# Attention and two mixture layers on one core: a product moved to VectorE, rows moved inside SBUF, grouped spreads

## The chip, the cores and the metric

The program runs on one core of a Trainium2 chip. The metric is the device time of one execution in microseconds (us). The engines are TensorE (PE, weight loads PEld), VectorE (DVE), ScalarE (ACT), GpSimd (POOL) and SyncE (SP, which here only issues DMAs).

## The reference, cut to what matters

```python
# B, H, S, D = 2, 8, 768, 40: attention over q, k, v with gates
m_new = np.maximum(f_gate[:, :, t] + m, i_gate[:, :, t])
C = f_stab * C + i_stab * einsum('bhd,bhe->bhde', vt, kt)
n = f_stab * n + i_stab * kt
y[:, :, t] = sigmoid(o_gate[:, :, t]) * einsum('bhde,bhe->bhd', C, qt) / maximum(abs(n . qt), 1)
# x = y as (1536, 320) rows, then a dense layer
h = x @ w_in                       # 320 -> 2048
g = maximum(h, 0) + log1p(exp(-abs(h)))
x = g @ w_out                      # 2048 -> 320
# then each token goes through its best one of 8 experts
h = maximum(x[mask] @ w1[e], 0); out[mask] = gate_w * eom * (h @ w2[e])
```

## The kernel before, in words

The order of the work is written out by hand: each engine has a block of its own with waits on semaphores, and every DMA but the gates' second half, the token fetches and the results is issued by SP, in one order.

**Attention, 16 heads in 8 pairs.** Time is cut into 6 chunks of 128 steps. For pair j (batch 0 is pairs 0 to 3, batch 1 pairs 4 to 7) TensorE broadcasts gate rows over the partitions (`cast`, L1382), computes the scores of keys and queries within a chunk (`scores`, L1407), the state updates of each chunk from `kw` and `v1` (`updates`, L1421), and the outputs, first from weighted scores `p_w` and `v1`, then from the states and `qd` (`outputs`, L1435). ScalarE copies casts out of PSUM (L803) and the finished pair to `stage` (L820). VectorE scans the forget gates over 768 steps, once per head (`scan`, L1071), scans the states (`states`, L1081), and multiplies scores by the decay (`weigh`, L1092). GpSimd makes `v1` = v times input gate (`inputs`, L610), `kw` = k times decay (`keys`, L622) and `qd` = q times decay (`queries`, L632). `v1` has 2 buffers, `kq` (keys and queries, 40 + 40 partitions) 3.

**Between attention and the dense layer.** A finished pair is stored to HBM (`store_pair`, L380: two times 40 rows to `attn_rows`, two normaliser rows to `nq_rows`). For batch 0 the rows come back early, heads 0 to 5 after pair 2 (`load_early`, L388), the rest after pair 3 (`load_late`, L396): `den` is the normaliser, 48 numbers to each partition, `xn` the output rows in three tiles of 128 partitions (tile 2 holds the last 64 rows twice). VectorE computes 1/max(|n.q|, 1) (`normaliser`, L1094); SP stores it to `rden_rows` and spreads it with one broadcast DMA for each piece of a head (`spread_normaliser`, L421) to `rb`. Then the tiles are multiplied by the output gate (`first_gate` L1103 on VectorE, `output_gate` L635 on GpSimd) and by `rb` (`normalise`, L1108), and split in a high part `xhi` (ScalarE, `high_part`, L827) and a low part `xlo` (VectorE, L1118). On VectorE the gate and `normalise(0)` stand between `states(6)` and `weigh(7)`.

**Dense layer, two batches of 16 tiles.** Each tile of `w_in` is loaded (L440), split in high and low on VectorE (`high_in`, L1139) and GpSimd (`split_in`, L668), multiplied in `hidden` (L1514: per half, for each 128 rows of x, high by high, high by low, low by high), goes through the softplus on ScalarE (L886) and VectorE (`gate_tile`, L1150), and through `second` (L1535). The first `hidden` waits for each tile's high and low part in turn. Batch 1's rows take the same way through HBM while batch 0's dense tiles run: its normaliser is spread after the third pair of tile loads (L503), in one queue with the loads of w_in and w_out. Afterwards come routing and the experts; the change does not touch them.

```python
for k, at, first, n in NORM_PIECES:
    if first_head <= first < last_head:
        sp.dma_start(rb[at:at + n, k, :], rden_rows[H * b + first:H * b + first + 1, :].to_broadcast([n, S])).then_inc(loaded, 16)
```

Of the kernel before, what the change touches and what calls it, by code (L numbers as in the profile page):

```python
# [6 lines left out]
ALU = mybir.AluOpType  # L7
# [8 lines left out]
P = 128  # L16
B, H, S, D = 2, 8, 768, 40
HEADS = B * H
NC = S // P
# [25 lines left out]
CONSTS = 17  # L45
# [21 lines left out]
NORM_PIECES = norm_pieces()  # L67
LATE_PIECES = sum(first >= EARLY for _, _, first, _ in NORM_PIECES)
EARLY_PIECES = len(NORM_PIECES) - LATE_PIECES
# [28 lines left out]
def build_program(nc, kq_t, k_rows, v_rows, o_t, gates, w_in, w_out, w_out_t, route_w, w1_e, w2_e, out):  # L98
    ctx = ExitStack()
    with ctx:  # L100
# [35 lines left out]
        need_k = keep.place("need_k", [P, TT], F32)  # L136
        table = keep.place("table", [P, TABLES, SLOTS + 1], I32)
# [19 lines left out]
        pick_1 = gat.place("pick_1", [P, HEADS], F32)  # L157
        assert gat.at <= after_x
# [17 lines left out]
        route_t = early.place("route_t", [P, F1 // 4], F32)  # L176
# [7 lines left out]
        v1 = [att.place(f"v1{u}", [P, 2 * NC, V1], F32) for u in range(2)]  # L184
# [81 lines left out]
        attn_rows = nc.dram_tensor("attn_rows", [HEADS * D, S], F32, kind="Internal").ap()  # L266
        nq_rows = nc.dram_tensor("nq_rows", [HEADS, S], F32, kind="Internal").ap()
# [16 lines left out]
        q_zeroed = sem("q_zeroed")  # L284
# [38 lines left out]
        block = ctx.enter_context(nc.Block())  # L323

# [39 lines left out]
        def _(sp):  # L364
            def load_kq(j):
                if j >= 3:
                    sp.wait_ge(scores_ready, j - 2)
                    sp.wait_ge(qd_done, j - 2)
                for h in range(2):
                    sp.dma_start(kq[j % 3][HALF * h:HALF * h + D, :, :], kq_t[2 * j + h].rearrange("d (k t) -> d k t", k=2)).then_inc(kq_loaded[j % 3], 16)  # L370
# [17 lines left out]
            def load_early():  # L388

                sp.wait_ge(stage_stored[0], 96)  # L390
                sp.wait_ge(stage_stored[1], 48)
                sp.dma_start(den[0:16 * EARLY, 0, :], nq_rows[0:EARLY, :].rearrange("h (p n) -> (h p) n", n=NQ)).then_inc(nq_early, 16)
                sp.dma_start(xn[:, 0, :], attn_rows[0:P, :]).then_inc(xn_early, 16)
                sp.dma_start(xn[0:EARLY * D - P, 1, :], attn_rows[P:EARLY * D, :]).then_inc(xn_loaded, 16)

            def load_late():  # L396

                sp.wait_ge(stage_stored[1], 96)
                sp.dma_start(den[16 * EARLY:P, 0, :], nq_rows[EARLY:H, :].rearrange("h (p n) -> (h p) n", n=NQ)).then_inc(nq_loaded, 16)
                sp.dma_start(xn[EARLY * D - P:P, 1, :], attn_rows[EARLY * D:2 * P, :]).then_inc(xn_loaded, 16)  # L400
                for at in (0, HALF):
# [1337 lines left out]
```

## Time and profile before

| what | us |
|---|---|
| median of 3 runs (420.04 to 422.71) | 420.82 |
| the profiled execution | 417.85 |
| its span, from the first to the last instruction | 416.1 |
| TensorE busy | 386.2 (93%) |
| VectorE busy | 283.7 (68%) |
| ScalarE busy | 225.9 (54%) |
| GpSimd busy | 212.2 (51%) |

The span is the profiled execution without its start and end. A timeline row gives start, duration, engine, line, operation, tiles and shapes, a count where several were merged, and in brackets the idle time before it and what ended that.
### The profile page before, as it was taken

How to read it: one execution, taken by the hardware profiler on the slowest of the kernel's cores; microseconds unless marked ns; L12 is line 12 of the kernel's file. 1: busy time of each engine (PE TensorE's matmuls, PEld its weight loads, DVE VectorE, ACT ScalarE, POOL GpSimd, SP SyncE). 2: the span in 40 equal slices, each digit the busy share in tenths (PEclk: the TensorE clock that was granted, in tenths of full speed). 3: DMA queues.
4: the chain of work that ended last, by engine and by line, in shares of the span. 5: the costliest groups of instructions: out<-in, count | busy, mean ns of one | idle time of the engine just before them, and what ended most of it. 6: DMA issues, size and time to landing. Idle time of an engine off the chain costs nothing.

```text
span 416.1 us, 9463 instructions
## 1 busy us (share of the span) xinstructions
PE 386.2 (93%) x2741; PEld 359.5 (86%) x2742; DVE 283.7 (68%) x496; ACT 225.9 (54%) x406; POOL 212.2 (51%) x225
## 2 busy tenths in 40 slices
PE   0999996899999999999999999599999999999983
PEld 0858886789999999999999999588998999899873
DVE  8999989958656788557766676677473257874231
ACT  4647772454556545655555655546465358874230
POOL 6577978436556665342434464045264423886221
PEclk9999997899999999999999999989999999999998
DMA  7979774335255544644222254225736219741110
GB/s 198 304 286 320 231 221 147 112 83 165 76 182 172 184 134 153 189 135 166 72 71 61 66 202 143 105 64 174 277 117 260 64 40 354 262 153 36 56 36 26
DMA packets 30682, 63.43 MB, mean 152 GB/s; under 512 B 8984, under 2 KB 20763, under 8 KB 30012
## 3 DMA queue, kind: packets, MB, share of 16 engines
q1 hardware_dynamic: 28780, 57.61, 42.6%
q0 software_dynamic: 1808, 5.31, 3.8%
q8 instruction: 14, 0.23, 0.2%
q10 hardware_dynamic: 64, 0.15, 0.1%
q14 instruction: 16, 0.13, 0.1%
HBM read 56.40 MB, written 6.88 MB: 152 GB/s over the span
## 4 chain that ended last, share of the span: by engine, by line
PE 83%; DVE 8%; issue 2%; DMA 2%; ACT 2%; DVEq 0%; POOL 0%; SPq 0%; POOLq 0%; ACTq 0%
PE ps L1541 7%; PE ps L1543 7%; PE ps L1542 7%; PE ps L1525 5%; PE ps L1527 5%; PE ps L1526 5%; PE ps L1674 4%; PE ps L1676 4%; PE ps L1675 4%; PE ps L1631 3%; PE ps L1633 3%; PE ps L1632 3%; PE ps L1658 3%; PE ps L1532 3%; PE ps L1533 3%
## 5 line engine op out<-in xcount | busy, mean ns | idle before, releaser
L1156 DVE SCALAR_TENSOR_TENSOR gsum<-ps,soft 128x384 f32<-128x384 f32 x64 | 35.7, 557 | 51.8 <-ACT soft L897 51.5
L670 POOL TENSOR_TENSOR win_lo<-win_raw,win_hi 128x256 fp32r<-128x256 f32 x32 | 25.1, 783 | 85.6 <-DVE win_hi L1143 85.6
L889 ACT ACTIVATE soft<-ps 128x384 f32<-128x384 f32 x64 | 31.5, 492 | 68.5 <-PE ps L1533 68.4
L1541 PE MATMUL ps<-wout_hi,ghi 128*128 128x336 f32 x192 | 61.1, 318 | 1.0 <-DVE glo L1162 1.0
L1542 PE MATMUL ps<-wout_lo,ghi 128*128 128x336 f32 x192 | 60.7, 316 | 0.0
L1543 PE MATMUL ps<-wout_hi,glo 128*128 128x336 f32 x192 | 60.7, 316 | 0.0
L1525 PE MATMUL ps<-xhi,win_hi 128*128 128x384 f32 x128 | 43.6, 341 | 0.8 <-DVE gsum L1156 0.8
L1527 PE MATMUL ps<-xhi,win_lo 128*128 128x384 f32 x128 | 43.3, 338 | 0.0
L1526 PE MATMUL ps<-xlo,win_hi 128*128 128x384 f32 x128 | 43.2, 338 | 0.0
L1674 PE MATMUL ps<-split,hthi 128*128 x120 | 38.3, 319 | 1.9 <-DVE htlo L1333 1.9
L737 POOL DMA_INDIRECT out<-yout,token x15 | 17.7, 1177 | 41.3 <-DVE yout L1341 40.3
L1541 PEld LDWEIGHTS ps<-wout_hi,ghi 128*128 128x128 f32 x192 | 36.1, 188 | 1.8 <-issue 1.2
L1676 PE MATMUL ps<-split,htlo 128*128 x120 | 37.1, 309 | 0.0
L1675 PE MATMUL ps<-split,hthi 128*128 x120 | 37.0, 308 | 0.0
L1542 PEld LDWEIGHTS ps<-wout_lo,ghi 128*128 128x128 f32 x192 | 36.2, 189 | 0.0
L1543 PEld LDWEIGHTS ps<-wout_hi,glo 128*128 128x128 f32 x192 | 36.2, 188 | 0.0
L710 POOL TENSOR_TENSOR split<-e2raw,split (+1 forms) x16 | 26.4, 1667 | 18.6 <-ACT split L946 15.7
L1159 DVE CAST ghi<-gsum 128x384 fp32r<-128x384 f32 x64 | 34.1, 575 | 0.0
L897 ACT ACTIVATE soft<-soft 128x384 f32<-128x384 f32 x64 | 33.4, 521 | 1.0
L893 ACT ACTIVATE soft<-soft 128x384 f32<-128x384 f32 x64 | 33.3, 521 | 1.0
L1071 DVE TENSOR_TENSOR_SCAN d_w<-f_all,ident 128x768 f32<-128x768 f32 x16 | 32.5, 2071 | 0.4 <-ACT f_all L803 0.3
L1162 DVE TENSOR_TENSOR glo<-gsum,ghi 128x384 fp32r<-128x384 f32 x64 | 32.5, 548 | 0.0
(214 smaller groups left out, 996.2 us busy)
## 6 DMA issues: line engine op xcount, KB each, us to landing
e1raw<-w_e SPq DMA_DIRECT2D x24, 512.0 KB
e2raw<-w_e SPq DMA_DIRECT2D x16, 640.0 KB, 5.2
win_raw<-w_in SPq DMA_DIRECT2D x32, 192.0 KB, 2.6
wout_raw<-w_out SPq DMA_DIRECT2D x32, 160.0 KB, 2.1
kq<-kq_t SPq DMA_DIRECT2D x16, 240.0 KB
wout_t<-w_out_t SPq DMA_DIRECT2D x3, 1024.0 KB, 14.1
og<-o_t SPq DMA_DIRECT2D x2, 1152.0 KB, 7.4
kr<-k_rows SPq DMA_DIRECT2D x8, 240.0 KB, 4.7
```

Of the source, the lines that this page charges most:

```text
L897: nc.scalar.activation(soft_half(f, hf), soft_half(f, hf), ACT.Ln, bias=1.0).then_inc(ln_done, 1)
L1156: dve.scalar_tensor_tensor(half(gsum, hf), ps[:, hf, 0:S // 2], 0.0, half(soft, hf), ALU.max, ALU.add).then_inc(g_done, 1)
L1159: dve.tensor_copy(half(ghi[u], hf), half(gsum, hf)).then_inc(ghi_done, 1)
L1525: pe.matmul(o, hi[:, k, :], xhi[b][:, k, cols], start=(k == 0), stop=False)
L1526: pe.matmul(o, hi[:, k, :], xlo[b][:, k, cols], start=False, stop=False)
L1527: pe.matmul(o, lo[:, k, :], xhi[b][:, k, cols], start=False, stop=False)
L1541: pe.matmul(o, ghi[u][:, cols], wout_hi[u][:, :], start=False, stop=False, skip_group_check=True)
L1542: pe.matmul(o, ghi[u][:, cols], wout_lo[u][:, :], start=False, stop=False, skip_group_check=True)
L1543: last = pe.matmul(o, glo[u][:, cols], wout_hi[u][:, :], start=False, stop=last_tile, skip_group_check=True)
L1674: pe.matmul(o, hthi[:, k, :], w(e2hi, k), start=(k == 0), stop=False)
L1675: pe.matmul(o, hthi[:, k, :], w(e2lo, k), start=False, stop=False)
L1676: last = pe.matmul(o, htlo[:, k, :], w(e2hi, k), start=False, stop=(k == FET - 1))
```

## The change

- `queries` (qd) moves from GpSimd to VectorE, behind the two scans and ahead of `weigh`; GpSimd waits for it before `keys` and `inputs`. `v1` gets a third buffer.
- Batch 0's rows are no longer stored and loaded: `store_pair` moves the normaliser row (16 partitions of 48) into `den` and the rows into `xn`, straight from `stage` in SBUF. Batch 1 keeps the way through HBM for its rows, but not for the normaliser. `load_early` and `load_late` go.
- `spread_normaliser` takes neighbouring whole heads together in one DMA: heads 0 to 2 (120 partitions), heads 4 and 5 (80 partitions). 9 DMAs for a batch in place of 12.
- VectorE gates tiles 0 and 2 (`open_tile`), GpSimd tile 1. ScalarE makes the high part of w_in's tile 0 after pair 4 and GpSimd its low part there.
- The first dense product (`first_hidden`) takes all products with `xhi` for both halves first and those with `xlo` last.
- Of VectorE's clears at the start, two of `kq` go to ScalarE and `f_start` to GpSimd.

```diff
+def head_pieces(head):
+    pieces = []
+    first, last = head * D, head * D + D
+    for k in range(KT):
+        lo, hi = max(first, k * P), min(last, k * P + P)
+        if lo < hi:
+            pieces.append((k, lo - k * P, lo - first, hi - lo))
+            if k == KT - 1:
+                pieces.append((k, lo - k * P + REM, lo - first, hi - lo))
+    return pieces
+
+def spreads(first_head, last_head):
+    groups = []
+    for k, at, head, n in norm_pieces():
+        if first_head <= head < last_head:
+            same = groups and n == D and groups[-1][4] == D and groups[-1][0] == k and groups[-1][1] + groups[-1][3] * D == at
+            if same:
+                groups[-1] = (k, groups[-1][1], groups[-1][2], groups[-1][3] + 1, D)
+            else:
+                groups.append((k, at, head, 1, n))
+    return groups
...
-        v1 = [att.place(f"v1{u}", [P, 2 * NC, V1], F32) for u in range(2)]
+        v1 = [att.place(f"v1{u}", [P, 2 * NC, V1], F32) for u in range(3)]
...
+        def wait_stored(engine, j):
+            engine.wait_ge(stage_stored[j % 2], STORED[j])
+
+        def wait_queries(engine, j):
+            engine.wait_ge(qd_done, j + 1)
...
             def store_pair(j):
...
                 for h in range(2):
-                    sp.dma_start(attn_rows[(2 * j + h) * D:(2 * j + h + 1) * D, :], stage[u][HALF * h:HALF * h + D, :]).then_inc(stage_stored[u], 16)
-                sp.dma_start(nq_rows[2 * j:2 * j + 2, :], stage[u][D:D + HALF + 1:HALF, :]).then_inc(stage_stored[u], 16)
+                    at = 16 * (2 * j + h - H * b)
+                    sp.dma_start(den[at:at + 16, b, :], stage[u][HALF * h + D:HALF * h + V1, :].rearrange("o (p n) -> o p n", n=NQ)).then_inc(stage_stored[u], 16)
+                for h in range(2):
+                    if b == 0:
+                        for k, at, first, n in head_pieces(2 * j + h):
+                            rows = slice(HALF * h + first, HALF * h + first + n)
+                            sp.dma_start(xn[at:at + n, k, :], stage[u][rows, :]).then_inc(stage_stored[u], 16)
+                    else:
+                        sp.dma_start(attn_rows[(2 * j + h - H) * D:(2 * j + h - H + 1) * D, :], stage[u][HALF * h:HALF * h + D, :]).then_inc(stage_stored[u], 16)
...
-                for k, at, first, n in NORM_PIECES:
-                    if first_head <= first < last_head:
-                        sp.dma_start(rb[at:at + n, k, :], rden_rows[H * b + first:H * b + first + 1, :].to_broadcast([n, S])).then_inc(loaded, 16)
+                for k, at, head, heads, n in spreads(first_head, last_head):
+                    source = rden_rows[H * b + head:H * b + head + heads, :]
+                    sp.dma_start(rb[at:at + heads * n, k, :],
+                                 source.unsqueeze(1).to_broadcast([heads, n, S])).then_inc(loaded, 16)
...
             for j in range(1, PAIRS - 1):
-                queries(j)
+                wait_queries(pool, j)
                 keys(j + 1)
                 inputs(j + 1)
+                if j == 5:
+                    split_in(0, 0)
+                    pool.wait_ge(win_split, 2)
...
             iteration(4)
+            act.wait_ge(win_loaded[0], 16)
+            nc.scalar.copy(win_hi[0][:, :, :], win_raw[0][:, :, :]).then_inc(win_hi_done, 1)
...
+            def open_tile(k):
+                for j in ((0, 1), (1, 2, 3), (3,))[k]:
+                    wait_stored(dve, j)
+                dve.wait_ge(og_ready, k + 1)
+                dve.tensor_tensor(xn[:, k, :], xn[:, k, :], og[0][:, k, :], ALU.mult).then_inc(z_first, 1)
...
                 if j == 4:
-                    normaliser(0, slice(0, 16 * EARLY), nq_early, 16, 0)
+                    normaliser(0, slice(0, 16 * EARLY), (1, 2), 0)
                 if j == 5:
-                    normaliser(0, slice(16 * EARLY, P), nq_loaded, 16, 1)
+                    normaliser(0, slice(16 * EARLY, P), (3,), 1)
+                queries(j + 1)
                 weigh(j + 1)
...
+            def first_hidden():
+                pe.wait_ge(win_split, 2)
+                pe.wait_ge(p_done, 2 * PAIRS)
+                hi, lo = win_hi[0], win_lo[0]
+                half = lambda hf: slice(hf * (S // 2), (hf + 1) * (S // 2))
+                for k in range(KT):
+                    pe.wait_ge(xhi_done, k + 1)
+                    for hf in range(2):
+                        o = ps[:, hf, 0:S // 2]
+                        pe.matmul(o, hi[:, k, :], xhi[0][:, k, half(hf)], start=(k == 0), stop=False, skip_group_check=True)
+                        if k < 2:
+                            pe.matmul(o, lo[:, k, :], xhi[0][:, k, half(hf)], start=False, stop=False, skip_group_check=True)
+                for hf in range(2):
+                    o = ps[:, hf, 0:S // 2]
+                    for k in range(KT):
+                        if hf == 0:
+                            pe.wait_ge(xlo_done, k + 1)
+                        last = pe.matmul(o, hi[:, k, :], xlo[0][:, k, half(hf)], start=False, stop=(k == KT - 1), skip_group_check=True)
+                    last.then_inc(h_ready, 1)
```

VectorE before, from pair 6's states to the low parts (`state`: chunk states, `p_w`: weighted scores, `og`: output gate, `rb`: spread normaliser):

```order
L1081 SCALAR_TENSOR_TENSOR state0_123<-carry0_121,ps 128x205 [waits pv_done,carry_done,update_ready]
L1143 CAST win_hi0_84<-win_raw0_80 128x384 [waits h_ready,win_loaded0]
L1106 TENSOR_TENSOR xn_129<-xn_129,og0_127 128x768 [waits og_ready,xn_early]
L1116 TENSOR_TENSOR xn_129<-xn_129,rb_130 128x768 [waits rb_early,z_first]
L1092 TENSOR_TENSOR p_w1_118<-ps,d_w1_116 128x768 [waits scan_done,pv_done,scores_ready]
L1092 TENSOR_TENSOR p_w1_118<-ps,d_w1_116 128x768 [waits scan_done]
L1081 SCALAR_TENSOR_TENSOR state1_124<-carry1_122,ps 128x205 [waits pv_done,carry_done,update_ready]
L1116 TENSOR_TENSOR xn_129<-xn_129,rb_130 128x768 [waits rb_loaded,rb_early,z_done]
L1120 TENSOR_TENSOR xlo0_69<-xn_129,xhi0_67 128x768 [waits xhi_done]
L1116 TENSOR_TENSOR xn_129<-xn_129,rb_130 128x768 [waits rb_loaded,rb_early,z_done]
L1120 TENSOR_TENSOR xlo0_69<-xn_129,xhi0_67 128x768 [waits xhi_done] x2
```

The same place on VectorE after the change (L1120 is `states`, L1156 `open_tile`, L1166 `normalise`, L1140 `queries`, L1131 `weigh`, L1170 `low_part`):

```order
L1120 SCALAR_TENSOR_TENSOR state0_125<-carry0_123,ps 128x205 [waits pv_done,carry_done,update_ready]
L1156 TENSOR_TENSOR xn_131<-xn_131,og0_129 128x768 [waits og_ready,stage_stored1,stage_stored0]
L1156 TENSOR_TENSOR xn_131<-xn_131,og0_129 128x768 [waits og_ready,stage_stored1]
L1166 TENSOR_TENSOR xn_131<-xn_131,rb_132 128x768 [waits rb_early,z_first]
L1140 TENSOR_TENSOR qd1_116<-kq1_102,d_all1_114 128x768 [waits pv_done,cast_read,kq_loaded1]
L1131 TENSOR_TENSOR p_w1_120<-ps,d_w1_118 128x768 [waits scan_done,pv_done,scores_ready]
L1131 TENSOR_TENSOR p_w1_120<-ps,d_w1_118 128x768 [waits scan_done]
L1120 SCALAR_TENSOR_TENSOR state1_126<-carry1_124,ps 128x205 [waits pv_done,carry_done,update_ready]
L1166 TENSOR_TENSOR xn_131<-xn_131,rb_132 128x768 [waits rb_loaded,rb_early,z_done]
L1166 TENSOR_TENSOR xn_131<-xn_131,rb_132 128x768 [waits rb_loaded,rb_early,z_first]
L1170 TENSOR_TENSOR xlo0_70<-xn_131,xhi0_68 128x768 [waits xhi_done] x3
```

The weight cast has gone, a second gate product and `queries` of pair 7 have come in, and `normalise(0)` still stands ahead of pair 7's `queries` and `weigh`.

SP's queue before, from the key loads of pair 7 to pair 4's store (`stage` to `attn_rows`):

```order
L377 DMA kr1_104<-k_rows 128x480 [waits v1_ready,kw_done]
L378 DMA vr1_106<-v_rows 128x480
L418 DMA rden_rows<-rden_132 96x48 [waits rden_done]
L399 DMA den_131<-nq_rows 32x48 [waits stage_stored1]
L400 DMA xn_129<-attn_rows 16x768
L402 DMA xn_129<-attn_rows 64x768 x2
L425 DMA rb_130<-rden_rows 40x768 [waits rden_early]
L425 DMA rb_130<-rden_rows 40x768 x2
L425 DMA rb_130<-rden_rows 8x768
L425 DMA rb_130<-rden_rows 32x768
L425 DMA rb_130<-rden_rows 40x768 x2
L385 DMA attn_rows<-stage0_125 40x768 [waits num_done]
```

The same place in SP's queue after the change (L455 stores the normaliser, L462 spreads it, L433 and L440 are `store_pair`):

```order
L424 DMA kr1_105<-k_rows 128x480 [waits v1_ready,kw_done]
L425 DMA vr1_107<-v_rows 128x480
L455 DMA rden_rows<-rden_134 96x48 [waits rden_done]
L462 DMA rb_132<-rden_rows 120x1x768 [waits rden_early]
L462 DMA rb_132<-rden_rows 8x1x768
L462 DMA rb_132<-rden_rows 32x1x768
L462 DMA rb_132<-rden_rows 80x1x768
L455 DMA rden_rows<-rden_134 32x48 [waits rden_done]
L433 DMA den_133<-stage0_127 16x1x48 [waits num_done]
L433 DMA den_133<-stage0_127 16x1x48
L440 DMA attn_rows<-stage0_127 40x768 x2
```

The four loads of batch 0's rest are gone, seven early spreads have become four, one of 120 and one of 80 partitions among them, and the second normaliser's store follows them directly.

## Rows read from the trace of the kernel before

**Rows 1.** Windows by stage: busy us (count) by engine, TensorE clock, DMA share, GB/s.

```profile
30.00:50.00 20.00, 20.00 (x310) 17.38 (x305) 18.30 (x16) 14.84 (x31) 17.75 (x13) 1.00 0.84 290
...
150.00:260.00 110.00, 109.94 (x668) 109.13 (x668) 74.97 (x174) 63.24 (x127) 48.62 (x62) 1.00 0.41 129
```

**Rows 2.** Timeline of TensorE: start, duration, operation, count, idle before and its end.

```profile
46.90 1.61 PE L1405 MATMUL ps<-kq 40*128 40x128 f32 x24
...
53.43 1.61 PE L1405 MATMUL ps<-kq 40*128 40x128 f32 x24
...
65.00 0.63 PE L1396 MATMUL ps<-d_parts,pick 128*128 128x256 f32 x3
68.92 2.93 PE L1405 MATMUL ps<-kq 40*128 40x128 f32 x24 [3.28 <-DVE p_w L1092]
...
77.63 1.51 PE L1444 MATMUL ps<-p_w,v 128*41 128x128 f32 x24 [0.99 <-ACT stage L820]
...
85.63 0.45 PE L1525 MATMUL ps<-xhi,win_hi 128*128 128x384 f32 x1 [0.76 <-DVE gsum L1156]
```

**Rows 3.** Timeline of VectorE, a quiet pair and the last two pairs.

```profile
25.54 3.41 DVE L1071 TENSOR_TENSOR_SCAN d_w<-f_all,ident 128x768 f32<-128x768 f32 x2
...
30.59 0.57 DVE L1081 TENSOR_TENSOR_SCAN state<-carry,ps 128x205 f32<-128x205 f32 x1
...
60.39 5.16 DVE L1071 TENSOR_TENSOR_SCAN d_w<-f_all,ident 128x768 f32<-128x768 f32 x2
...
66.94 1.82 DVE L1092 TENSOR_TENSOR p_w<-ps,d_w 128x768 f32<-128x768 f32 x2
...
70.09 2.56 DVE L1106 TENSOR_TENSOR xn<-xn,og 128x768 f32<-128x768 f32 x1
72.68 2.45 DVE L1116 TENSOR_TENSOR xn<-xn,rb 128x768 f32<-128x768 f32 x1
...
78.13 0.94 DVE L1120 TENSOR_TENSOR xlo<-xn,xhi 128x768 fp32r<-128x768 f32 x1
```

**Rows 4.** Timeline of GpSimd in the last two pairs.

```profile
61.02 2.92 POOL L632 TENSOR_TENSOR qd<-kq,d_all 128x768 f32<-128x768 f32 x1 [0.31 <-issue]
...
71.80 2.52 POOL L639 TENSOR_TENSOR xn<-xn,og 128x768 f32<-128x768 f32 x1
```

**Rows 5.** Timeline of SP's DMA issues: the normaliser's store and its spreads.

```profile
58.67 0.42 SPq L418 DMA_DIRECT2D rden_rows<-rden  x1
...
65.47 2.72 SPq L425 DMA_DIRECT2D rb<-rden_rows  x7
...
73.03 1.89 SPq L425 DMA_DIRECT2D rb<-rden_rows  x5
...
114.20 4.61 SPq L425 DMA_DIRECT2D rb<-rden_rows  x12
```

**Rows 6.** DMA issues from 58 to 60 us: size, us from issue to landing.

```profile
rden_rows<-rden SPq DMA_DIRECT2D x1, 18.0 KB, 5.8
```

**Rows 7.** Windows of half a microsecond, columns as in rows 1.

```profile
55.50:56.00 0.50, 0.50 (x11) 0.36 (x10) 0.31 (x1) 0.50 (x2) 0.50 (x1) 1.00 1.10 424
67.50:68.00 0.50, 0.00 (x0) 0.00 (x0) 0.50 (x2) 0.15 (x1) 0.00 (x0) 1.00 0.64 246
71.00:71.50 0.50, 0.50 (x8) 0.50 (x6) 0.50 (x1) 0.00 (x0) 0.50 (x1) 0.50 0.64 253
74.50:75.00 0.50, 0.50 (x9) 0.50 (x6) 0.50 (x1) 0.00 (x0) 0.50 (x1) 0.55 0.68 191
```

**Rows 8.** Timeline of ScalarE: the first softplus half.

```profile
82.57 0.49 ACT L889 ACTIVATE soft<-ps 128x384 f32<-128x384 f32 x1 [1.06 <-PE ps L1533]
```

**Rows 9.** Timelines behind the late spreads: VectorE's and GpSimd's split, TensorE's next tile.

```profile
122.70 0.36 DVE L1143 CAST win_hi<-win_raw 128x384 fp32r<-128x384 f32 x1 [1.68 <-DMA win_raw<-w_in]
...
123.98 0.46 POOL L674 TENSOR_TENSOR win_hi<-win_raw,win_hi 64x128 fp32r<-64x128 f32 x1
...
124.87 0.34 PE L1525 MATMUL ps<-xhi,win_hi 128*128 128x384 f32 x1
```

More of the change, by code:

```diff
@@ L64, in norm_pieces, with stage_counts @@
     return pieces
-NORM_PIECES = norm_pieces()
-LATE_PIECES = sum(first >= EARLY for _, _, first, _ in NORM_PIECES)
-EARLY_PIECES = len(NORM_PIECES) - LATE_PIECES
+def head_pieces(head):
[18 more added lines that the diff above has]
+    return groups
+EARLY_SPREADS, LATE_SPREADS, ALL_SPREADS = len(spreads(0, EARLY)), len(spreads(EARLY, H)), len(spreads(0, H))
+def stage_counts():
+    counts, so_far = [], [0, 0]
+    for j in range(PAIRS):
+        stores = 2 + (sum(len(head_pieces(2 * j + h)) for h in range(2)) if 2 * j < H else 2)
+        so_far[j % 2] += 16 * stores
+        counts.append(so_far[j % 2])
+    return counts
+STORED = stage_counts()
 def casts_of(j):
@@ L674, in split_in @@
                 pool.tensor_tensor(win_hi[u][low, 2, :], win_raw[u][low, 2, :], win_hi[u][low, 2, :].bitcast(F32), ALU.subtract).then_inc(win_split, 1)
+            pool.wait_ge(const_pool, CONSTS)
+            pool.wait_ge(istab_ready, 1)
+            inputs(0)
+            pool.wait_ge(scan_done, 2)
+            keys(0)
+            inputs(1)
+            wait_queries(pool, 0)
+            keys(1)
+            for j in range(1, PAIRS - 1):
+                wait_queries(pool, j)
+                keys(j + 1)
+                inputs(j + 1)
+                if j == 5:
+                    split_in(0, 0)
+                    pool.wait_ge(win_split, 2)
+            wait_queries(pool, PAIRS - 1)
+            output_gate(0, 1)
             def split_out(f, u, more=True):
@@ L773, in _ @@
             act.preload_act_table_set("natural_log_exp_and_others")
+            act.wait_ge(zero_ready, 1)
+            for u in range(1, 3):
+                nc.scalar.copy(kq[u][:, 1, :], zero_1[:, :].to_broadcast([P, S])).then_inc(q_zeroed[1], 1)
             act.wait_ge(pick_1_done, 1)
@@ L1092, in weigh, with queries, normaliser @@
                     dve.tensor_tensor(p_w[u][:, h, :], banks(0, 3, 2 * S)[:, h * S:(h + 1) * S], d_w[u][:, h, :], ALU.mult).then_inc(p_done, 1)
-            def normaliser(b, rows, loaded, count, before):
-                dve.wait_ge(loaded, count)
+            def queries(j):
+                u = j % 2
+                dve.wait_ge(kq_loaded[j % 3], 32 * (j // 3) + 32)
+                dve.wait_ge(cast_read, D_CAST[j])
+                if j >= 2:
+                    dve.wait_ge(pv_done, j - 1)
+                dve.tensor_tensor(qd[u][:, :], kq[j % 3][:, 1, :], d_all[u][:, :], ALU.mult).then_inc(qd_done, 1)
+            def normaliser(b, rows, pairs, before):
+                for j in pairs:
+                    wait_stored(dve, j)
                 dve.tensor_scalar(rden[rows, b, :], den[rows, b, :], -1.0, 1.0, ALU.mult, ALU.max).then_inc(den_done, 1)
@@ L1128, in _ @@
                 scan(1, h)
+            queries(0)
             for j in range(PAIRS - 2):
@@ L1176, in _ @@
             states(PAIRS - 2)
-            high_in(0, 0, 16)
-            first_gate()
+            open_tile(0)
+            open_tile(2)
             normalise(0)
+            queries(PAIRS - 1)
             weigh(PAIRS - 1)
@@ L1197, in _ @@
             tiles(0)
[L1198 removed]
+            normaliser(1, slice(0, P), (6, 7), 2)
             with dve.Fori(1, FT // 2) as i:
```

161 lines of the change are left out of this document (61 added, 100 removed).

## The prediction

> **What bounds the kernel now.** I read the windows by stage first. From 150 to 260 us TensorE is busy 109.94 of 110 us, 0.165 us for each of its 668 matmuls; the dense products up to there are bound by TensorE and are left alone by the change. In the attention pairs, 30 to 50 us, TensorE is also full, and VectorE, at 18.30 of 20, is close behind [rows 1]. What a change of the other engines can win lies between the pairs and the dense loop. TensorE's timeline shows it. A pair takes 6.53 us (46.90 to 53.43). After pair 7's casts end at 65.63 TensorE waits 3.28 us for `weigh(6)`, then runs the scores in 2.93 us where 1.61 was the rule, then waits 0.99 us more, and the second dense tile starts at 85.63 after 0.76 us [rows 2]. The granted clock explains the 2.93: it stands at 0.50 (1.2 GHz) at 71.0 and is back at 1.00 (2.4 GHz) at about 74.7 [rows 7], some six microseconds after TensorE resumed, behind an idle time of 3.28 us; the idle 0.99 us later brought no such slow row.
>
> VectorE's timeline says why `weigh(6)` was late. Two scans take 3.41 us when GpSimd rests (25.54) and 5.16 at 60.39; multiply-and-gate operations of 0.94 us take 2.56 and 2.45 at 70.09 and 72.68 [rows 3]. In each case GpSimd has a two-operand product in hand, and these stretch too: 2.92 at 61.02, 2.52 at 71.80 [rows 4]. 61.02 + 2.92 = 63.94, and from there to the end of the scans at 65.55 is 1.6 us, just one scan. So one waits for the other to finish. The Trainium skill (SBUF — State Buffer, Who interferes with whom) says the same of a VectorE instruction with two SBUF inputs against a GpSimd one that reads SBUF, and adds that the loser blocks entirely. By it GpSimd's early split of tile 0, which lands on scan(7), delays `weigh(6)` by its whole length of 0.8 us; if the two only shared, by half of it.
>
> **The parts, one by one** (times on this execution's scale: 417.85 us with 416.1 of span).
>
> *Clears off VectorE.* VectorE's scan of the gates starts at 4.5 us after the gate load; its clears had ended before. Gain 0; between -0.3 and +0.2. ScalarE's two copies fit before the `pick` it owes at 11 us.
>
> *Product q times d on VectorE.* VectorE per pair: scans 3.41, `weigh` 1.82, state 0.57, new product 0.94 (the row at 78.13 is the same shape) [rows 3], 6.7 less 0.1 where one starts before the last has ended: 6.4 to 6.7 us against TensorE's 6.53. GpSimd keeps `kw` and `v`, some 2 us, and is now made to wait for the product, so they fall under `weigh` and the state, which read PSUM. In the full pairs the gain is 0, bounds -0.5 to +1. At the end it counts: scan(7) runs in 3.41 instead of 5.16, the normaliser before it no longer waits for a trip through HBM, and `weigh(6)` ends near 66.5 to 67.5 instead of 68.77, GpSimd's early split of tile 0 included. TensorE then idles 1 to 2 us instead of 3.28, and keeps its clock: 1.4 + (2.93 - 1.61) + about 1.5 for the updates and outputs behind at half clock = 4.2 us by the time `outputs(6)` ends (near 72.4). The third v buffer only lets GpSimd's `v` start earlier; no row of v ends a TensorE wait, so 0.
>
> *Rows moved inside SBUF.* Four to seven short DMAs per pair take the place of three, and the loads of the same rows from HBM go. SP issues a DMA in 0.33 to 0.5 us; the store of the first normaliser, at 58.67 before [rows 5], moves to about 59.7, behind the seven DMAs of pair 3. It took 5.8 us to land [rows 6]; with 240 rows of 3 KB less in the queue I take 64.4, bounds 62 to 65.5.
>
> *First dense product, high parts first.* 16 matmuls of 0.165 us, 2.6 us as before; only the low parts are waited for later. Alone it gives up to 1.5 us, since the second half needs no wait of its own.
>
> *Spreads grouped.* Before, a head's 40 rows were one DMA. While only 40-row DMAs are in flight the mean busy share is 0.64, at 246 and 253 GB/s; with 128-row ones it is full at 424 GB/s [rows 7]. 0.64 of 16 is 10 engines, four rows each; one engine moves 24.6 GB/s. The division seen follows the outermost count of the pattern. The new source pattern is [3 heads, 40 times the same row, 768] and [2 heads, 40, 768], so its outermost count is 3 and 2. No row shows such a pattern; the bounds are ten engines as now (120 rows in 1.5 us) and three (368 KB at 74 GB/s, 5.0 us), then two for the next (245 KB at 49 GB/s, 5.0 us). I take three and two, since the row nearest to it divides by the outermost count and not by the rows in all. All DMAs start at the first engines, if the shares add as I think, so engine 0 has 83 of the early rows, 255 KB: 10.4 us. The Trainium skill (DMA: Bandwidth & Descriptors, Why a DMA increments its semaphore by 16 and not by 1) states that the number of engines is the largest up to 16 that divides the slowest dimension above one on both sides; the 40-row plateau agrees, and no run here shows 3. By it the early spreads end at 75.5, and by ten engines for all rows near 68.5.
>
> **Early consequence.** First spread out at 64.4, all landed at 75.5. `normalise(0)` stands ahead of `queries(7)` and `weigh(7)` on VectorE, so they queue behind: 75.5 + 0.9 + 0.9 + 1.8 = 79.1. TensorE, idle since 72.4, is over the 3.28 us that cost it the clock before. Its 44 matmuls of `outputs(7)`, 2.8 us at full clock (1.51 x 44/24 [rows 2]), take about 4.8, to 83.9. The late normaliser's store and spreads wait behind the same engines (76, then 79.5) and `normalise(1)`, `normalise(2)` and three low parts end near 84. Then 16 matmuls, a quarter of them slow: 87.2, the first half at 86.8. From the first h_ready at 82.5 before (ScalarE's 82.57 [rows 8]) to TensorE's 85.63 it was 3.1 us; less 0.4, as both halves come together: 89.5. Loss against 85.63: 3.8 us with these values; 1.6 if the store lands at 62 and the clock returns sooner. I take 2.9.
>
> **Late consequence.** Batch 1's spreads go out in the midst of the dense loop, at 114.20 [rows 5]. Engine 0 then has 96 rows, 295 KB: 12.0 us, to 127.2, and the next input weights wait behind them: 127.7. Before, VectorE waited 1.68 us for these and cast them at 122.70; TensorE used them at 124.87, with GpSimd's split, ending at 124.44, between [rows 9]: slack 0.4. Stall 127.7 - 122.7 - 0.4 = 4.6 us, 3.7 with engines at 26.5 GB/s (424/16). An idle time beyond 3.28 us cost six microseconds at half clock, 3 us of work; so 3.7 to 7.6. I take 5.7.
>
> Sum: 2.9 + 5.7 = 8.6 us slower, 426.4 for the profiled execution. The median of the runs shown, 420.82, stands 3.0 above the profiled one, so 429.4 on the runs' scale; own range 424.5 to 432.5.
>
> **The rivals.**
> 1. *The grouped spreads use ten engines or more.* Then the early rows land by about 68.5 and `weigh(7)` ends near 73.2, `normalise(1)` follows the late spreads at 74.6 (issued 1 us sooner than 73.03 [rows 5]), low parts at 79, h_ready at 79.2, the next tile at 79.2 + 2.7 = 82: 3.5 us faster, up to 5.3 if DMAs land sooner. For it: SP issues fewer DMAs, and the gain of `weigh(6)` stands in any case. Against it: nothing shown divides by the product of the counts. 420.82 - 3.5 = 417.3, range 415.5 to 419. It decides from the point where the early spreads land before 69, when `normalise(0)` is ready.
> 2. *The order on VectorE gives the gain back.* Spreads of ten engines, but the first store takes its 5.8 us, the spreads land near 70 to 71, `weigh(7)` starts after 73, TensorE's idle time passes 3.28 us and the half clock costs 2 to 3 us. Result between -1 and +1: 421. Against it: 40-row spreads landed in time before.
> 3. *Narrow early, harmless late*: the weights of batch 1 are asked for 1.2 us sooner and the stall is under 2 us. 420.82 + 2.9 + 1 = 424.7. The 0.4 us of slack speaks against it.
>
> **Chances.** Forecast 0.50, rival 1 0.30, rival 2 0.10, rival 3 0.10. About 1%, 4.2 us, is what a measurement of this kernel can tell from no change. Rival 1 is faster by more than that in half of its range: 0.15. Within 1%: the other half, rival 2 and half of rival 3: 0.30. Slower: 0.55. The range, 416.5 to 432.5, leaves out the best of rival 1 and the worst of two full stalls.
>
> **What would show it.** Right: a DMA share of about 0.2 (3 of 16) for some microseconds after the first spreads near 65 and again after 114; VectorE's `normalise(0)` waiting on a DMA to about 75; high_in waiting 4 to 6 us near 123 to 128; the clock at 0.50 behind both. VectorE's scans in pairs of 3.4 us up to the last, and no TensorE wait of 3.28 us at 65.6, in every case. Wrong: share 0.6 or more in the spreads, `normalise(0)` without a wait, the second dense tile at 82; then the grouping is free and the kernel is faster. If the pairs take over 6.6 us, the product on VectorE costs what I called nothing.

## The result, and the profile after

The changed kernel takes 437.02 us (433.42 to 438.23, 4 runs) where the kernel before took 420.43 beside it: ratio 1.0358, 95% interval 1.0307 to 1.0410. That is 16.6 us slower; 8.6 were predicted, and the time lies outside the predicted range. Medians are over all runs of a kernel, ratios and their intervals over its fast runs. The profiled execution is 438.23 us with 436.4 of span, 20.3 more span than before.

The windows by stage of the changed kernel; read them against [rows 1], the columns are the same:

```profile
30.00:50.00 20.00, 19.59 (x291) 16.89 (x291) 20.00 (x20) 14.93 (x30) 8.60 (x9) 1.00 0.86 276
50.00:70.00 20.00, 17.60 (x271) 15.44 (x273) 18.41 (x23) 11.60 (x24) 9.62 (x12) 0.98 0.47 140
70.00:90.00 20.00, 13.19 (x126) 11.24 (x125) 8.64 (x11) 3.89 (x5) 1.81 (x1) 0.59 0.29 92
130.00:150.00 20.00, 12.46 (x62) 12.19 (x61) 6.06 (x14) 5.79 (x13) 6.01 (x7) 0.74 0.47 147
150.00:260.00 110.00, 109.95 (x671) 109.66 (x670) 73.07 (x175) 63.47 (x127) 49.56 (x62) 1.00 0.40 120
```

Two stretches lose the time, 70 to 90 and 130 to 150 us: TensorE is idle for a third and more of each, and its granted clock is 0.59 and 0.74 on the mean. The dense loop behind them is what it was. TensorE's timeline, to be read with [rows 2], says when:

```profile
50.82 0.70 PE L1484 MATMUL ps<-v,kw 128*40 128x41 f32 x17 [1.24 <-issue]
68.80 2.63 PE L1457 MATMUL ps<-kq 40*128 40x128 f32 x24 [1.58 <-DVE p_w L1131]
83.67 2.79 PE L1496 MATMUL ps<-p_w,v 128*41 128x128 f32 x24 [6.81 <-DVE p_w L1131]
...
92.05 1.69 PE L1599 MATMUL ps<-xlo,win_hi 128*128 128x384 f32 x6
95.83 0.45 PE L1574 MATMUL ps<-xhi,win_hi 128*128 128x384 f32 x1 [1.17 <-DVE gsum L1208]
142.69 0.68 PE L1574 MATMUL ps<-xhi,win_hi 128*128 128x384 f32 x1 [7.54 <-POOL win_hi L692]
```

The second dense tile starts at 95.83 where it was 85.63: 10.2 us, half of the 20.3, are lost by then. The other half goes in one stall of 7.54 us that ends at 142.69, and in the half clock after it. GpSimd is named there, but it had only waited for VectorE, and VectorE for a transfer. VectorE's timeline at the same places, for [rows 3] and [rows 9]:

```profile
60.10 3.87 DVE L1110 TENSOR_TENSOR_SCAN d_w<-f_all,ident 128x768 f32<-128x768 f32 x2
65.03 0.18 DVE L1146 TENSOR_SCALAR rden<-den 32x48 f32<-32x48 f32 x1 [1.06 <-DMA xn<-stage]
66.84 1.81 DVE L1131 TENSOR_TENSOR p_w<-ps,d_w 128x768 f32<-128x768 f32 x2
80.06 0.96 DVE L1166 TENSOR_TENSOR xn<-xn,rb 128x768 f32<-128x768 f32 x1 [9.19 <-DMA rb<-rden_rows]
86.27 1.83 DVE L1166 TENSOR_TENSOR xn<-xn,rb 128x768 f32<-128x768 f32 x2 [2.16 <-DMA rb<-rden_rows]
88.01 2.69 DVE L1170 TENSOR_TENSOR xlo<-xn,xhi 128x768 fp32r<-128x768 f32 x3
140.85 0.36 DVE L1195 CAST win_hi<-win_raw 128x384 fp32r<-128x384 f32 x1 [9.70 <-DMA win_raw<-w_in]
```

`normalise(0)` waits 9.19 us for the early spreads, `normalise(1)` again for the late ones, and in the dense loop the cast of input weights waits 9.70 us where it was 1.68. SP's issues of the changed kernel, for [rows 5], and its second store of the normaliser, for [rows 6] (last line: 10.7 us from issue to landing):

```profile
59.00 3.77 SPq L438 DMA_DIRECT2D xn<-stage  x5
64.16 0.42 SPq L455 DMA_DIRECT2D rden_rows<-rden  x1
66.66 2.77 SPq L462 DMA_DIRECT2D rb<-rden_rows  x4
80.16 3.59 SPq L462 DMA_DIRECT2D rb<-rden_rows  x5
124.36 6.72 SPq L462 DMA_DIRECT2D rb<-rden_rows  x9
131.22 0.39 SPq L480 DMA_DIRECT2D win_raw<-w_in  x1
...
rden_rows<-rden SPq DMA_DIRECT2D x1, 6.0 KB, 10.7
```

Two things stand out. The second store, 6 KB, lands 10.7 us after its issue (in e1, the ungrouped version below, it landed in 3.3): it is queued behind the spreads. And a spread takes SP 0.7 to 0.75 us to issue, where twelve took 4.61 before, 0.38 each. The narrow transfer itself shows in the windows of the two stalls, when little but spreads is in flight, and in 0.9 us behind the first late spread, the one of three heads:

```profile
76.00:78.00 2.00, 0.86 (x16) 0.62 (x12) 0.00 (x0) 0.00 (x0) 0.00 (x0) 1.00 0.13 52
78.00:80.00 2.00, 0.00 (x0) 0.00 (x0) 0.00 (x0) 0.00 (x0) 0.00 (x0) 0.85 0.12 48
136.00:138.00 2.00, 0.00 (x0) 0.00 (x0) 0.00 (x0) 0.00 (x0) 0.00 (x0) 0.86 0.13 50
138.00:140.00 2.00, 0.00 (x0) 0.00 (x0) 0.00 (x0) 0.00 (x0) 0.00 (x0) 0.50 0.13 48
...
126.20:127.10 0.90, 0.90 (x7) 0.90 (x6) 0.00 (x0) 0.55 (x2) 0.74 (x3) 1.00 0.19 75
```

A share of 0.13 is 2 of 16 engines, and 50 GB/s is twice the 24.6 GB/s of one engine that the prediction worked out from [rows 7]. A share of 0.19 is 3 of 16, and 75 GB/s is three times that.

### The profile page after: what moved, and what is told of

It is laid out like the page before. It is cut to its first block, busy times and chain, and to the rows that moved or that the text cites. A ratio compares the mean times of both kernels' runs of the same rounds, so it can differ in the third digit from the quotient of the medians.

```text
span 436.4 us, 9466 instructions
## 1 busy us (share of the span) xinstructions
PE 390.4 (89%) x2741; PEld 363.1 (83%) x2742; DVE 275.1 (63%) x501; ACT 227.9 (52%) x409; POOL 184.6 (42%) x218
## 4 chain that ended last, share of the span: by engine, by line
PE 71%; DMA 9%; issue 7%; POOL 3%; SPq 3%; ACT 3%; DVE 2%; POOLq 0%; DVEq 0%; ACTq 0%
PE ps L1608 5%; PE ps L1610 5%; PE ps L1609 5%; PE ps L1741 4%; PE ps L1574 4%; PE ps L1743 4%; PE ps L1742 4%; PE ps L1576 4%; PE ps L1575 4%; DMA wout_t<-w_out_t 3%; PE ps L1698 3%; PE ps L1700 3%; PE ps L1699 3%; PE ps L1725 3%; DMA rb<-rden_rows 3%
## 5 line engine op out<-in xcount | busy, mean ns | idle before, releaser
L1208 DVE SCALAR_TENSOR_TENSOR gsum<-ps,soft 128x384 f32<-128x384 f32 x64 | 35.6, 558 | 59.8 <-ACT soft L937 59.7
L1574 PEld LDWEIGHTS ps<-xhi,win_hi 128*128 128x128 f32 x124 | 23.8, 192 | 9.3 <-DVE gsum L1208 9.3
L716 POOL TENSOR_TENSOR wout_lo<-wout_raw,wout_hi 128x336 fp32r<-128x336 f32 x32 | 29.2, 913 | 4.6 <-DVE wout_hi L1200 1.8
```

What stands on the lines that cost most here:

```text
L1208: dve.scalar_tensor_tensor(half(gsum, hf), ps[:, hf, 0:S // 2], 0.0, half(soft, hf), ALU.max, ALU.add).then_inc(g_done, 1)
L1574: pe.matmul(o, hi[:, k, :], xhi[b][:, k, cols], start=(k == 0), stop=False)
```

## The experiments

**The grouping alone.** Theory A is the forecast's: the grouped spreads run on 3 and 2 engines. Theory B is SP's longer time for an issue, theory C the order on VectorE. Four kernels divide the change at that edit. In e1 the function issues one head at a time, in the old form:

```diff
-                    sp.dma_start(rb[at:at + heads * n, k, :],
-                                 source.unsqueeze(1).to_broadcast([heads, n, S])).then_inc(loaded, 16)
+                    sp.dma_start(rb[at:at + n, k, :], source.to_broadcast([n, S])).then_inc(loaded, 16)
```

> The changed kernel with every head's spread as a DMA of its own again, source pattern [rows, 768] as before, in both batches; all else as changed. Theory A (the grouped spreads run on 3 and 2 engines, and that makes both stalls): normalise(0)'s wait of 9.2 us and high_in's of 9.7 us go, the clock stays up behind them; only the 1.7 us lost in the pairs remain and the gain at weigh(6): 418 to 422 us, ratio to before about 1.00. Theory B (SP is late because its DMAs are slower to issue, 0.7 us where 0.35 were the rule, and the first store leaves 5.5 us later): ungrouping makes 12 issues out of 9, helps by less than 6 us: 430 to 435. Theory C (order on VectorE: normalise(0) ahead of weigh(7) costs by itself, whatever the width of the spreads): late stall goes, early one stays at 4 to 5 us: 424 to 427.

Measured: 417.79 us, ratio 0.9929 (0.9891 to 0.9966). In e2 only batch 1's spreads are grouped, in e3 only batch 0's:

> Batch 0's spreads one head each, batch 1's grouped as in the change. Theory A: the late stall alone, some 10 us above the kernel with both ungrouped: 429 to 432. Theory B: little from batch 0's width, 433 to 437. Theory C: 433 to 436, since the early loss isn't the width's.

> Batch 0's spreads grouped, batch 1's one head each. Theory A: the early stall alone, 8 to 9 us above the kernel with both ungrouped: 426 to 430. Theory B: 430 to 435. Theory C: 427, the same as the kernel with both ungrouped to within 2 us.

Measured: 425.26 us for the late ones (ratio 1.0129, 1.0059 to 1.0198) and 427.38 for the early ones (1.0201, 1.0109 to 1.0293): 7.5 and 9.6 us above e1. The second is rough: without the longest of its four runs, 431.70, the median is 425.56, 7.8 above e1. e4 puts the function `spreads` into the kernel before and changes nothing else:

> The kernel before with nothing changed but the grouping of the spreads, both batches. Theory A: nearly the whole loss of the change, 8 to 10 us late and 6 to 9 us early (the first normaliser lands as early as before, so the early part may be smaller): 434 to 440. Theory B: the issue of the spreads themselves is 0.7 us each but there are fewer, so no change within 2 us: 419 to 423. Theory C: 419 to 425.

Measured: 437.07 us, ratio 1.0387 (1.0320 to 1.0454), the time of the whole change: alone, the grouping costs 16 us against the kernel before, and 19 between e1 and the change. Theory A's ranges hold e3 and e4, and e1 but for 0.2 us; e2 is 3.7 us faster than A's range, so A had the late part too large. B misses all four; C's 427 meets e3 as a number, but not what C says, that e3 equals e1. All other edits of the change together are worth 0.7% by e1's ratio, 3 us faster. In e1 both waits are gone (SP's issues, then VectorE's timeline):

```profile
66.11 2.50 SPq L469 DMA_DIRECT2D rb<-rden_rows  x7
112.24 4.61 SPq L469 DMA_DIRECT2D rb<-rden_rows  x12
```

```profile
71.83 0.96 DVE L1172 TENSOR_TENSOR xn<-xn,rb 128x768 f32<-128x768 f32 x1 [1.44 <-DMA rb<-rden_rows]
121.29 0.36 DVE L1201 CAST win_hi<-win_raw 128x384 fp32r<-128x384 f32 x1 [2.07 <-DMA win_raw<-w_in]
```

**Count or form?** e6 leaves one head to a DMA, and only writes the source with a small outermost count:

```diff
-                    sp.dma_start(rb[at:at + n, k, :], source.to_broadcast([n, S])).then_inc(loaded, 16)
+                    sp.dma_start(rb[at:at + n, k, :],
+                                 source.unsqueeze(1).to_broadcast([n // 8, 8, S])).then_inc(loaded, 16)
```

> The kernel with both batches ungrouped (e1: 417.8 us), with each head's spread still a DMA of its own, 12 for a batch, but its source pattern written as [rows / 8, 8 times the row, 768], so that the outermost count is 5 for a head of 40 rows (4, 3, 2 for the shorter pieces). No heads are grouped. Theory A (the outermost count sets the number of engines, and the first engines carry every such DMA): the first engine gets 49 early rows where grouping gave it 83 and one head each about 23, and 89 late rows where grouping gave 96: 6.1 and 11.1 us of its time by 24.6 GB/s. So an early loss of about 3.5 us and a late one of 6 to 7: 426 to 429. DMA share near 0.31 (5 of 16) while only spreads are in flight. Rival D (it is the DMA over several heads, one source row after another, that is slow, not its count): no change against e1, 416 to 420.

Measured: 434.14 us, ratio 1.0328 (1.0258 to 1.0397). So no grouping of heads is needed for the loss, and rival D falls. The mean DMA share while its late spreads run is 0.31, 5 of 16:

```profile
121.00:131.00 10.00, 10.00 (x63) 10.00 (x62) 4.42 (x11) 5.67 (x12) 3.94 (x4) 1.00 0.31 97
```

But the time is 5 to 8 us above what A's rows of the first engine give, and SP's row points at a reason: 9.05 us for 12 issues at 121.26. e10 keeps that form without any small count:

```diff
-                    sp.dma_start(rb[at:at + n, k, :], source.to_broadcast([n, S])).then_inc(loaded, 16)
+                    sp.dma_start(rb[at:at + n, k, :],
+                                 source.unsqueeze(1).to_broadcast([1, n, S])).then_inc(loaded, 16)
```

> e1 (one head each, 417.8 us) with only the source's form changed, from [n rows, 768] to [1, n rows, 768]: the same rows, the same 12 DMAs of a batch, no count of 2, 3 or 5 in it, but three dimensions, as the change writes them. The kernel by eights lost 6 us more than its first engine's rows explain, and its spreads took SP 0.75 us each instead of 0.36. If the form costs SP its time and nothing else: issues of 5.2 and 9.0 us for 7 and 12 DMAs, mean DMA share while they go about 0.4 instead of 0.64, the next input weights asked for 4.4 us later than in e1, so a late stall of 3 to 6 us: 422 to 426. If only the number of engines counts (here still ten): 417 to 419. If a leading 1 confines the DMA to one engine: 120 KB at 24.6 GB/s, 5 us for each, 440 us or more.

Measured: 426.00 us, ratio 1.0129 (1.0057 to 1.0201), 8.2 us above e1 for a leading 1 in the pattern. Some of that may be chance: in the profiled execution TensorE waited 1.23 us before 50.34, ran at half clock to 53 us, and the first spread went out 1.5 us later than in e1. Its SP and VectorE timelines, and a window in the midst of the late spreads:

```profile
67.64 5.00 SPq L465 DMA_DIRECT2D rb<-rden_rows  x7
117.50 8.68 SPq L465 DMA_DIRECT2D rb<-rden_rows  x12
```

```profile
75.32 0.96 DVE L1169 TENSOR_TENSOR xn<-xn,rb 128x768 f32<-128x768 f32 x1 [3.38 <-DMA rb<-rden_rows]
129.10 0.36 DVE L1198 CAST win_hi<-win_raw 128x384 fp32r<-128x384 f32 x1 [4.75 <-DMA win_raw<-w_in]
```

```profile
119.00:124.00 5.00, 5.00 (x32) 5.00 (x31) 2.53 (x7) 2.52 (x6) 3.77 (x4) 1.00 0.48 143
```

SP takes 0.72 us an issue, twice the 0.36 to 0.38 of the plain form. A share of 0.48 can't be 1, 2 or 5 engines; ten engines that are busy 0.5 us (four rows of 3 KB each) out of every 0.72 give 0.43. So, by the share, this form has the width of the old one and only its price at SP. e6 has the same form and the same number of DMAs as e10 and differs only in the counts: 434.14 against 426.00, 8.1 us for the narrow engines, with SP's time nearly the same (9.05 and 8.68 us). That is the clearest evidence for theory A; the change itself is 11.0 us above e10. The rule of the Trainium skill that the prediction cited (DMA: Bandwidth & Descriptors, Why a DMA increments its semaphore by 16 and not by 1) passes over a count of one, and this run agrees.

One measure for all kernels, from SP's and VectorE's timelines: the time from the first spread's issue to the first operation that waited for it or for what stood behind it.

| kernel | engines | to `normalise(0)` | batch 1: SP busy with spreads | to the cast of the next input weights |
|---|---|---|---|---|
| e1, one head, plain form | 10 | 5.7 us | 4.6 us | 9.1 us |
| e10, [1, n, 768] | 10 | 7.7 | 8.7 | 11.6 |
| e6, [n / 8, 8, 768] | 5 and fewer | 9.9 | 9.1 | 15.9 |
| the change, grouped | 3, 2 | 13.4 | 6.7 | 16.5 |
| e3 (early) and e2 (late) | 3, 2 | 13.3 | 6.6 | 16.7 |

Against e10, grouping saves SP 2 us, and the next input weights are still ready 4.9 us later.

**The product on VectorE.** e7 is e1 with `queries` back on GpSimd in its old place:

```diff
-                queries(j + 1)
                 weigh(j + 1)
...
-                wait_queries(pool, j)
+                queries(j)
                 keys(j + 1)
```

> e1 with the product q times d back on GpSimd in its old place between v and kw, all else as in e1. The claim of the forecast (the product on VectorE gives scan(7) its 3.4 us back, the wait of TensorE for weigh(6) falls from 3.3 to 1.6 us, 2 to 4 us in all): 420 to 422, TensorE waits about 3 us for weigh(6) and the scans of 5 us are back. Rival (the product's place is worth nothing, e1's gain comes from the rows moved inside SBUF and the high parts first): 417 to 418.5.

Measured: 419.92 us, ratio 0.9996 (0.9956 to 1.0036): some 2.2 us slower than e1, at the edge of what the intervals part. TensorE waited 2.76 us for `weigh(6)` (1.66 in e1). So, as far as the two can be parted, most of e1's gain is the product's place, and the rows moved inside SBUF, the high parts first and the clears show no gain together.

**What holds pair 7.** From e1 I moved the second normaliser behind `weigh(6)` (e8), then also the first store ahead of pair 3's stores on SP (e9):

```diff
-                if j == 5:
-                    normaliser(0, slice(16 * EARLY, P), (3,), 1)
                 queries(j + 1)
                 weigh(j + 1)
+                if j == 5:
+                    normaliser(0, slice(16 * EARLY, P), (3,), 1)
...
+            store_normaliser(0, 0, EARLY, 1, rden_early)
             store_pair(3)
             load_rows(7)
-            store_normaliser(0, 0, EARLY, 1, rden_early)
```

> e1 with the second normaliser of batch 0 (three operations, 1.0 us, and 0.8 us of waiting for the rows of pair 3) moved behind queries(6) and weigh(6) on VectorE. If that wait and those operations are what TensorE's 1.66 us before scores(7) is made of, the idle time falls to about 0, the clock stays at full speed through outputs(6), and the second store leaves SP at the same time as it is queued behind the spreads: 414 to 416.5. If the rows of the normaliser are on the path to the low parts instead, the gain is given back: 417 to 419.

> e8 and, on SP's queue, the first store of the normaliser ahead of pair 3's seven stores in place of behind them and the row loads. The first rows of rb should land 2 us sooner, normalise(0) without its 1.4 us wait, the second store and its spreads 1 us sooner: 413.5 to 416. If SP's queue then delays pair 7's row loads so that updates(7) wait, the same as e8 or up to 1 us slower.

Measured: 420.01 us (0.9984, 0.9948 to 1.0019) and 418.13 (0.9957, 0.9921 to 0.9993), neither better than e1, and both above what I expected. The idle time before the scores at 67.50 had gone, but it came back some 6 us later, before outputs(7). TensorE in e8:

```profile
67.50 1.61 PE L1463 MATMUL ps<-kq 40*128 40x128 f32 x24
76.24 2.79 PE L1502 MATMUL ps<-p_w,v 128*41 128x128 f32 x24 [3.61 <-DVE p_w L1137]
```

`weigh(7)` stands behind `normalise(0)`. e11 moves it ahead in the change itself, e12 in e9:

```diff
-            normalise(0)
             queries(PAIRS - 1)
             weigh(PAIRS - 1)
             states(PAIRS - 1)
+            normalise(0)
```

> The change as it stands, spreads grouped, with queries(7), weigh(7) and states(7) ahead of normalise(0) on VectorE, so that pair 7 doesn't queue behind the first spreads. If the order makes the early loss, TensorE runs outputs(7) straight after outputs(6), the 6.8 us of idle time before them go, and 3 us or more are won: 431 to 434. If the spreads alone bound it (normalise(1) and (2) wait for the late ones to 86.3, and the low parts for these), TensorE waits the same time a little later, behind outputs(7): 435 to 438, within 1.5 us of the change.

> e9 (ungrouped, second normaliser behind weigh(6), first store early; 418.1 us) and pair 7's product and weigh ahead of normalise(0). The 2.1 us that TensorE waited for weigh(7) should go, and the clock with it stay up; but the low parts still end with the late spreads, so the second dense tile comes at most 0.5 us sooner: 416.5 to 418.5, not told apart from e1. If TensorE's idle time and half clock were the bound: 414 to 416.

Measured: 435.21 us (1.0316, 1.0244 to 1.0387), 1.8 below the change and inside its interval; and 420.48 (0.9977, 0.9940 to 1.0013), no better than e9 and above the 418.5 I had allowed. TensorE still idled before outputs(7), 5.94 us in the one and 3.84 in the other, and now it was ScalarE that released it: its copy of outputs(6) stood behind xhi(0), which waits for the same `normalise(0)`. e14 (from e11) and e13 (from e12) turn this round too:

```diff
-            high_part(0, 0)
             iteration(7)
-            for k in range(1, KT):
+            for k in range(KT):
                 high_part(0, k)
```

> The change with pair 7's product and weigh ahead of normalise(0) on VectorE, and on ScalarE the copy of outputs(6) to its stage ahead of the high part of tile 0. The kernel with VectorE's order alone won 1.8 us of 16.6; there TensorE still idled 5.9 us, ended by ScalarE's stage copy, which stood behind xhi(0) and with it behind the spreads. Theory E (the two narrow rounds of spreads bound the early stage by themselves: late ones landed at 86.3, then two products and three low parts to 90.7): TensorE's wait moves behind outputs(7) and stays as long, 434 to 437. Theory F (what costs is pair 7 behind them, with its half clock): outputs(7) run at 76.9 without a wait and 3 us or more go against the change: 430 to 433.5.

> Ungrouped, second normaliser behind weigh(6), first store early, pair 7's weigh ahead of normalise(0) (that kernel: 420.5 us, TensorE idle 3.8 us before outputs(7), ended by ScalarE's stage copy), and now the stage copy ahead of the high part of tile 0 on ScalarE. TensorE should then run outputs(7) from 73.4 and the first dense product as soon as xhi is there; the low parts end at 79.6, the second dense tile starts near 82.3 where 85.6 and 83.4 (e9) were measured: 415.5 to 418. If the clock falls all the same or something else is late: 418 to 421.

Measured: 435.40 us (1.0350, 1.0293 to 1.0407) with the change's spreads, and 416.73 (0.9928, 0.9895 to 0.9961) without. In the first, outputs(7) waited a third time, 6.37 us. ScalarE's row shows for what:

```profile
79.67 0.80 ACT L858 COPY stage<-ps 128x768 f32<-128x768 f32 x1 [11.73 <-DMA attn_rows<-stage]
```

The stage buffer was not free: pair 4's stores, issued behind the early spreads, had to wait for the same engines. Theory E holds as far as the time goes (no gain against the change); F stays untried, since in no kernel with grouped early spreads did outputs(7) run without a wait. e15 is e1 again, run beside these two:

> The same kernel as e1, beside the others on this chip. 417 to 419, ratio to before 0.99 to 0.996; a ratio of 1.00 would say that e1's gain of 0.7% was its chip's or the chance's.

Measured: 417.67 us, ratio 0.9947 (0.9916 to 0.9979). Its interval overlaps that of the version with all orders turned (e13), 0.9928, so e13 and e15 can't be told apart; both beat the kernel before by 0.5 to 0.7%. Turned orders took TensorE's idle time away one wait at a time, and the second dense tile still began at 83.35 us (83.90 in e1, 83.12 in e15). In e13 TensorE waited 0.43 us for the low parts, which stand behind the late spreads and ended at 80.2 (80.8 in e1).

## Why the prediction was right and wrong

**What failed.** The mechanism was right and the sizes of both terms of the sum 2.9 + 5.7 too small. The step that failed is the time for which the narrow spreads hold up what waits for them: 11.1 us taken early and 13.5 late, 13.4 and 16.5 measured. With it went the date of the first store and the length of the half clock. By the profiles the early part cost 10.2 us and the late one 10.0, of 20.3 in all; the medians are 16.6 us apart, as the profiled execution before, 417.85, was shorter than the runs beside it and the one after the longest of its four.

**Clears: no gain, as said.** VectorE's scan of the gates starts at 4.86 us (4.53 before), and in both kernels it waits for the gates' load.

**Product q times d: right in the pairs, wrong at their end.** The full pairs still take 6.53 us, the scans came in 3.87 at 60.10 (5.16 before), and TensorE's wait fell from 3.28 to 1.58 us, as predicted (1 to 2). The step that failed is "and keeps its clock": the scores after those 1.58 us took 2.63, and the granted clock stood at 0.50 from 70 to 76 us. (In the kernel before it was back at about 74.95, not 74.7: the last of [rows 7] has a mean of 0.55.) `weigh(6)` ended at 68.65 and not at 66.5 to 67.5, for two reasons. The first is a term with the wrong sign: I wrote that the normaliser ahead of `weigh(6)` "no longer waits for a trip through HBM". In the kernel before it had not waited at all there, and now it waits 1.06 us for the copies inside SBUF (65.03, above). In e8, with this normaliser behind `weigh(6)`, TensorE's wait is gone. Before:

```profile
65.58 0.34 DVE L1097 TENSOR_SCALAR rden<-den 32x48 f32<-32x48 f32 x1
```

The second is that pair 5 had slipped by 1.7 us. 1.24 of the slip is TensorE's wait at 50.82, for GpSimd, which had this to do:

```profile
45.34 3.71 POOL L662 TENSOR_TENSOR kw<-kr,d_w 128x200 f32<-128x200 f32 x2 [6.74 <-DMA vr<-v_rows]
49.02 1.70 POOL L650 TENSOR_TENSOR v<-vr,istab_t 128x480 f32<-128x480 f32 x1
```

GpSimd had waited for rows that SP had asked for behind pair 0's four copies, so `kw` fell under two scans: 3.71 us for what takes 1.02 alone. I had put `kw` and `v` at nothing, because they would lie under `weigh`. In e1 TensorE's wait there is 0.28 us and in e13 1.23, with the same copies, so its size differs by chance; I made no run for it.

**Rows inside SBUF: the first store mis-sized.** Issued at 64.16, not 59.7; landed in 2.5 us, not 4.7; the first spread at 66.66 and not 64.4. Of the 4.5 us to the issue 1.7 are the slip, and 2.8 the price of the seven DMAs ahead of it: 0.6 and 0.75 us each, where I had counted 0.33 to 0.5.

**High parts first: not tested alone.** In the change TensorE took the products with the low parts without a wait (92.05).

**Spreads grouped: the mechanism right, the term short.** Three and two engines, the share, both waits and both half clocks came as written. For the first engine's rows alone I had 10.4 us early and 12.0 late, and allowed 0.7 and 1.5 for all the rest; measured are 3.0 and 4.5. In it are SP's time, 0.7 us an issue, a start longer than I allowed (no DMA engine was busy from 66.5 to 68.0 us, behind the first spread's issue at 66.66), other transfers on the same engines and, late, the weights' own share of them. These are named from the rows and not parted by a run; that the form costs by itself is shown by e10.

**Early loss: 2.9 taken, 10.2 measured** (95.83 against 85.63). My own dates gave 89.5 and a loss of 3.8, of which I took less. From 89.5 to 95.83: the first spread went out 2.3 us later, the spreads lasted 2.3 longer, outputs(7) 0.3, and the first dense product ran wholly at half clock, 5.1 us from 88.68, where I had a quarter of it slow: 1.6 more to its first half. The second round of spreads was late too (used at 86.27, low parts at 90.7 where I had 84), but TensorE did not wait for it. Nor did the 4.2 us of missing gain count: TensorE's idle time began later (76.9 where I had 72.4) and ended with `weigh(7)`, which hangs on the spreads. Against the ungrouped kernel I had 2.9 + 3.5 = 6.4; e3 against e1 gave 9.6, or 7.8 without e3's longest run.

**Late loss: 5.7 taken, 7.5 measured** (e2 against e1), within the bounds 3.7 to 7.6. In the profile of the full change it is more: 7.54 us of idle time, where the stall was to be 4.6, and behind it a clock of 0.50 to 147.7 us, 5.0 us of matmuls at half speed, which costs 2.5.

**Rivals.** Rival 1 (ten engines, 417.3) is what e1 measured, 417.8, so its number stood and its condition didn't; in part by luck, since it had the second dense tile at 82 and e1's profile has it at 83.90. Rival 2 had the right queue and too small a part: with the order turned in the change, 1.8 us at most; the rank of the waits behind it (ScalarE's order, then the stage's stores) I hadn't seen. Rival 3, a harmless late part, falls: 7.5 us.

## What to carry to other kernels

Before merging DMAs, read the pattern's outermost count on both sides: fewer and larger DMAs can run on fewer engines, and here 12 spreads made into 9, twice, cost 16 to 19 us. Part of it is the narrow engines and everything that queued behind them there (8.1 us between e10 and e6), part SP's time for the form (8.2 us between e1 and e10). Keep a broadcast in two dimensions where it can be written so, and look at SP's time for one issue and not only at the count of issues. And where a wait is removed, follow the next one down each queue: the place of pair 7 hung in turn on VectorE's order, on ScalarE's, and on a buffer's stores.

## What the runs showed of the hardware that I had not expected

- The form of the source alone doubles SP's time: 0.36 to 0.38 us on the mean for a row broadcast as [n, 768], 0.72 for [1, n, 768], with the same rows and, by the share, the same engines.
- Copies of 16 to 40 rows from SBUF to SBUF took SP 0.75 us each (59.00), while stores of 40 rows from the same buffer to HBM took 0.44 (two in 0.88 us at 71.37).
- Idle times of 1.58 us and 1.66 us (e1) on TensorE were followed by a clock of 0.50 for some 7 and 3.5 us. Behind 1.24 us (50.82), 1.42 us (e13, before outputs(7)) and 1.53 us (e6, before 51.19) it stayed at 1.00, but 1.23 us in e10 (before 50.34) brought it down for 3.5 us. So the length of the last idle time alone does not tell.
- GpSimd's `kw` products stretch from 1.02 to 3.71 us under two scans of VectorE, and its early split of the input weights to 4.53 us in e8 (0.76 alone).
